# Products nobody reads, ahead of a kernel's prologue and behind each level's block in it

## What is computed

```python
# 1: 8 heads of 48 channels, a state of 48 x 48 per head
for t in range(S):
    cur = einsum('bhd,bhe->bhde', u * k_t, v_t)
    y[t] = einsum('bhd,bhde->bhe', r_t, state + cur)
    state = w_t[..., None] * state + einsum('bhd,bhe->bhde', k_t, v_t)
# 2: x is y as (4, 768, 384)
u  = x + (relu(x.T @ w_tok1) @ w_tok2).T          # mixing over tokens, 768 -> 256 -> 768
x2 = u + relu(u @ w_ch1) @ w_ch2                  # 384 -> 1536 -> 384
# 3
gate = sigmoid(causal 5-tap convolution of x2 along the tokens)
out  = (gate * (x2 @ w_val)) @ w_out              # 384 -> 384 -> 384
```

## Time and profile before

| | us |
|---|---|
| median of 3 runs | 733.45 |
| lowest and highest | 733.14, 733.71 |
| profiled execution | 737.69 |
| its span, first to last instruction | 736.0 |
| TensorE (PE) busy in the span | 680.0 |
| VectorE (DVE) busy | 407.7 |
| ScalarE (ACT), GpSimd (POOL) busy | 200.5, 102.4 |
| mean granted TensorE clock | 0.939 |

### The profile page before, as it was taken

How to read it: one execution, slowest core, us unless ns; L and a number is a source line. 1 busy time by engine, 2 the same in 40 slices (tenths; PEclk the granted TensorE clock), 3 DMA queues, 4 the chain that set the end, 5 groups by cost and what they waited for, 6 DMA issues and landing times.

```text
span 736.0 us, 26444 instructions
## 1 busy us (share of the span) xinstructions
PE 680.0 (92%) x12244; PEld 652.6 (89%) x12244; DVE 407.7 (55%) x624; ACT 200.5 (27%) x366; POOL 102.4 (14%) x139
## 2 busy tenths in 40 slices
PE   4558888999999999999999999999999999999995
PEld 3458878998989999989989999999989998999995
DVE  2749727639476548437485638429476534252524
ACT  2220340422423313311323313312323223131322
POOL 6121561130200200020210300030300100000000
PEclk9655578999999999998999999999999999999998
DMA  9594245250050320060050230040000000000000
GB/s 146 106 154 94 68 99 117 83 90 11 6 99 10 56 55 24 3 88 3 3 88 24 35 76 23 3 67 3 3 24 3 2 22 22 1 2 1 22 22 22
DMA packets 111357, 32.77 MB, mean 45 GB/s; under 512 B 104080, under 2 KB 110224, under 8 KB 111248
## 3 DMA queue, kind: packets, MB, share of 16 engines
q1 hardware_dynamic: 107792, 26.37, 21.0%
q10 hardware_dynamic: 3456, 4.72, 1.8%
HBM read 26.35 MB, written 4.72 MB: 42 GB/s over the span
## 4 chain that ended last, share of the span: by engine, by line
PE 69%; DVE 17%; SPq 4%; issue 4%; ACT 4%; DMA 1%; DVEq 0%; ACTq 0%
PE ps L733 66%; DVE gate L702 4%; DVE rk L572 4%; DVE at L625 3%; PE ps L755 3%; SPq L336 2%; SPq L323 2%; ACT x2s L454 1%; ACT gate L537 1%; DVE wp L572 1%; DMA nat<-in_k_dram 1%; DVE xf L679 1%; ACT hid L521 1%; DVE xf L683 1%; DVE us L664 1%
## 5 line engine op out<-in xcount | busy, mean ns | idle before, releaser
L733 PE MATMUL ps<-hid,ch 128*128 128x256 f32 x1296 | 172.1, 287 | 0.0
L733 PE MATMUL ps<-us,ch 128*128 128x256 f32 x1296 | 170.6, 286 | 1.5 <-DVE us L664 0.8
L733 PEld LDWEIGHTS ps<-us,ch 128*128 128x128 f32 x1296 | 160.0, 189 | 6.2 <-DVE us L664 2.0
L733 PEld LDWEIGHTS ps<-hid,ch 128*128 128x128 f32 x1296 | 160.9, 190 | 1.5
L651 DVE SCALAR_TENSOR_TENSOR hid<-ps,hid 128x512 fp32r<-128x512 f32 x72 | 50.0, 694 | 127.9 <-ACT hid L521 127.6
L572 DVE TENSOR_TENSOR rk<-rk,wp 112x1024 f32<-112x1024 f32 x72 | 89.6, 1244 | 45.3 <-PE ps L733 45.2
L733 PE MATMUL ps<-rk 48*64 48x32 f32 x4608 | 95.4, 237 | 19.1 <-DVE at L625 9.0
L733 PEld LDWEIGHTS ps<-rk 48*64 48x64 f32 x4608 | 88.3, 155 | 27.3 <-issue 13.4
L521 ACT ACTIVATE hid<-ps 128x512 fp32r<-128x512 f32 x72 | 42.8, 595 | 160.3 <-PE ps L733 160.3
L702 DVE SCALAR_TENSOR_TENSOR gate<-xf,cw,gate 128x256 f32<-128x256 f32 x144 | 74.7, 566 | 4.4 <-ACT gate L537 3.5
L625 DVE COPY_PREDICATED at<-mask,ps 128x512 f32<-128x512 uint8 x72 | 65.4, 908 | 0.0
(11 more groups left out here) (71 smaller groups left out, 619.1 us busy)
## 6 DMA issues: line engine op xcount, KB each, us to landing
nat<-in_r_dram SPq DMA_DIRECT2D x24, 192.0 KB, 4.0
nat<-in_k_dram SPq DMA_DIRECT2D x24, 192.0 KB, 5.0
nat<-in_w_dram SPq DMA_DIRECT2D x24, 192.0 KB, 5.1
vs<-in_v_dram SPq DMA_DIRECT2D x96, 48.0 KB, 2.5
out_dram<-gate ACTq DMA_DIRECT2D x24, 192.0 KB, 2.0
gate<-in_moe_w_ch_dram SPq DMA_DIRECT2D x6, 384.0 KB, 3.6
xf<-in_moe_w_ch_dram SPq DMA_DIRECT2D x6, 384.0 KB, 4.0
gate<-in_moe_w_tok_dram SPq DMA_DIRECT2D x2, 384.0 KB, 5.2
```

Of the source, the lines that this page charges most:

```text
L733: return nc.tensor.matmul(out, lhsT, rhs, start=start, stop=stop, skip_group_check=True, **kw)
```

## The change

A function `keep_clock` issues four products, one in each quarter of the array. Stationary is a 64x64 part of the identity matrix, moving are 128 of its columns, and the results go to columns 0 to 127 of banks 0 and 1, which hold nothing at that time: the first product of the dense stages writes there anew, after the last of them. It is called 16 times as soon as the identity matrix is there, ahead of the first transposes, and once behind every L block (six levels, not F) of super-units 0 to 2. These are 34 calls and 136 products. No wait and no increment is added or moved, and no other engine's work.

```diff
+IDLE_COLS, FIRST_IDLE = 128, 16
...
+            def keep_clock():
+
+                for two in range(2):
+                    for par in range(2):
+                        rows, turn = slice(par * CH, (par + 1) * CH), slot(par, 2 * two)
+                        mm(ps[turn * CH:(turn + 1) * CH, RING + par, 0:IDLE_COLS], ident[rows, 0:CH],
+                           ident[rows, 0:P].unsqueeze(1).to_broadcast([CH, IDLE_COLS // P, P]), True)
...
                     scores(s, bank, CH // 2, lambda rows, ph: r_sides[home(s)][rows, ph * CH:(ph + 1) * CH]
                            .rearrange("p (n two i) -> p n two i", two=2, i=m)[:, :, 1], lev_done[m])
+                    if s < SUPERS:
+                        keep_clock()
...
             pe.wait_ge(ident_done, 1)
+            for _ in range(FIRST_IDLE):
+                keep_clock()
```

## The result

| | before | change |
|---|---|---|
| median of 9 runs, us | 733.45 | 737.91 |
| lowest, highest | 732.93, 735.2 | 733.77, 740.58 |
| profiled execution, us | 737.69 | 738.54 |
| its span, us | 736.0 | 736.8 |

The ratio of the change to the kernel before is 1.0045, with a 95% interval from 1.0024 to 1.0065: slower, by 1.8 to 4.8 us. The medians stand 4.5 apart. The forecast was 3.9, at 737.3. Ratios leave out executions over 1.5% above the fastest of their kernel; of all kernels in this document only e3 had such executions, three of twelve.

A forecast was written before the change was run, and what follows sets the result against it. The prediction took the prologue as bound by SyncE's DMA issue, then mostly VectorE with TensorE even at half clock, then TensorE. Terms 1.0 + 2.4 + 0.5 gave 3.9 us slower, 737.3 us, range 730.0 to 740.5.

The forecast's parts named there:

- a delay at L16:2 arrives whole at the end: At VectorE's multiplication for L16:2, lag of 1.0 + 2.4 us arrives whole and is counted in full in the time.
- The signs named beforehand: Profile after: clock 0.50 from 52 to 97 us, saturated blocks 2.3 us apart, VectorE waiting from about 72, dense products about 4 later.
- The start costs nothing: 16 groups ahead of the first transposes, covered by SyncE's issue until 36.15 us and a load: nothing; 3 to 5 us uncovered.
- The two groups at 46 to 48: Two groups after the blocks at 46.3 to 48.3 us, where TensorE then has nothing until 52.2: no cost.
- Six groups, 1.0 us of lag: Between 52.2 and 67.3 us, 2.9 us of groups against 2.0 us of TensorE idle: 1.0 us lag, bounds 0 and 2.9.
- the gap would be swallowed by slower issue: A 0.82 us TensorE idle before 63.61 us, put down to issue, which slower issue may swallow.
- Five groups, 2.4 us: Behind the five saturated blocks, before T:0: 5 x 0.49 = 2.4 us; VectorE's lag soaks up the first three groups.
- The group behind L32:2, 0.5 us: The group after L32:2 stands in the stage where TensorE is the chain and costs 0.5 us.
- The cold case: The prologue's clock stays at half despite the groups: 3.9 us slower, 737.3 us, spread 735 to 740.5; chance 0.53.
- The reason I gave: Prologue clock: a group is only 0.49 of each 2.34 us, the rest being products of a kind that did not suffice.
- Rival 1: Groups lift the clock from some point after 52 us and hold it to 96: 3 us saved, 730.4 us; chance 0.25.
- Rival 3: A half-clock stretch in the dense part vanishes or appears, 3 to 5 us either way, on top of others; no separate chance.

The follow-up runs named there:

- e3: The change with groups of 512 columns in place of 128, 4 at the start and 18 behind blocks; ratio to the kernel before 1.0029.
- e5: Groups of 128 columns only behind the five blocks of the saturated stretch, none at the start; ratio to the kernel before 0.9979.
- e6: Groups of 128 columns only behind the six blocks ahead of the saturated stretch, none at the start; ratio to the kernel before 0.9960.
- e12: 24 groups at the start and none behind blocks; ratio to the kernel before 0.9994.
- e1: The change without the groups behind the blocks, only the 16 at the start; ratio to the kernel before 0.9997.
- e4: The change with groups of 32 columns in place of 128, 64 at the start and 18 behind blocks; ratio to the kernel before 1.0079.
- e2: The change without the groups at the start, only the 18 behind the blocks; ratio to the kernel before 1.0052.
- e10: The change with 22 groups at the start in place of 16, all 18 behind blocks kept; ratio to the kernel before 1.0043.
- e7: Groups of 512 columns only behind ten blocks from L2:2 to L32:2, none at the start; ratio to the kernel before 1.0101.

## Why the prediction was right, and where its sum was off

**Sign and size.** Slower by 3.9 us was forecast; 1.8 to 4.8 was measured. That the forecast lies so close is in part luck: of its terms one was too high, one cost was missing, and the step on which it rests, that a delay at L16:2 arrives whole at the end, failed in e5, e6 and e12. The runs show that the loss comes with the groups behind the blocks; by what path it reaches the end they do not show.

**The signs named beforehand.** The profiled execution was to come to 741.6 us and came to 738.54. The blocks stand 2.15 apart, not 2.3. VectorE was to be idle before its multiplications from about 72 us and waits from 79.64 on. The first dense product is 3.4 us late (116.59 against 113.18), where about 4 was said.

**The start costs nothing.** Right, by e1. The groups took 6.02 us rather than 7.8. With 64 groups (e4) the load came late, and the stage began 3.9 us later than before; whether through them is open.

**The two groups at 46 to 48.** Not run alone. In the change L4:1 follows an idle spell of 3.0 us (3.9 before), so they lie in idle time.

**Six groups, 1.0 us of lag.** In the profile of the change L4:2 starts 27.0 us behind the transposes, against 26.1 before (67.29 - 41.22): 1.0 us. In e2 it is 28.4, 2.3 more than before, beside issue gaps of 1.14 and 0.85 us inside L1:2 and L2:2 (the change has 0.58). In e6, which has these six alone, it is 26.7, 0.6 more, and VectorE's multiplication for L4:2 is not late at all. So the lag of TensorE was of the forecast's order. But VectorE's lateness at L4:2 (0.4 us in the change, 1.3 in e2, 2.2 in e10) goes with where the gaps of issue fall, and e12 has 1.9 without these groups. That the gap would be swallowed by slower issue held only in part.

**Five groups, 2.4 us.** Mis-sized. They cost 0.33 each, 1.6 in all. I scaled the length of the F block, 1.96 us from its first start to its last end, but what a block costs in a row of blocks is the distance to the next start. In the kernel before, the next block starts 1.74 us behind that F block (28.87):

```profile
30.61 1.88 PE L733 MATMUL ps<-rk 48*64 48x32 f32 x64
```

16/64 of 1.74 is 0.44, and 0.43 is what a group took alone. The further 0.1 is hidden behind a block: the weight loads of the next block start under the group's products (68.51, with the group at 68.26 to 69.03). The consequence stood in the change: VectorE's slack took up the first ones, and L16:2 came 2.4 us late in the change (3.4 forecast), 4.1 in e2 and 4.7 in e10.

**The group behind L32:2, 0.5 us.** VectorE's multiplication for L32:2 is 3.1 us late in the change (46.2 against 43.1 behind the transposes), so 0.6 was added already between L16:2 and L32:2, where I had nothing. It is made up of the multiplication for L16:2, 1.6 longer beside GpSimd's subtraction, and of L32:2's own products, ready 0.96 sooner with the short rise of the clock. In e2, without the rise, 1.1 was added there. What lies beyond L32:2 varies by more than this term from kernel to kernel, and it was not tested alone.

**The clock.** The cold case came: 0.50 from 52.2 to 76.5. After that it rose for 3.4 us, which shortened L32:2 by up to 0.96 and was then lost in the idle spell in T:1. The reason I gave, that the rest of the mix is of a kind that did not suffice, is weaker than it looked: that rise came with only small products and groups since 47 us, and in e3 the clock rose, in e7 it did not, with the same mix. Nor was it so that each rise before came with transposes or 128x384 products: the one at 336.0 us came with 128x256 products. The sentence of the Trainium skill ("TensorE: Matmul & The Clock Gate", "Why this matters for your kernels") that I set against the row fares as it did: TensorE busy 9.20 of 9.20 us at 0.50 again, and 9.00 of 9.00 in e7.

**Rival 1** was priced at 730.4 if the clock rose. e3 shows the full clock from 63 to 94 without that gain, though with wider groups; the time expected from the TensorE pieces of the chain went into gaps of issue. So the rival's price was too high where its condition was met. **Rival 3** is what separated the profiles: the half-clock stretch at 330 was there in one and not in the other.

**What was not foreseen:** that a few groups (e5, e6) leave the whole kernel no slower although they delay L16:2 by over 1 us. The chain from L16:2 to the dense work is looser than my sum had it, and a delay of 1 to 2 us there need not arrive. Whether it is the 2.4 to 4.7 us at L16:2 that arrive in the change, e2 and e10, or something else that the 18 groups bring, is open.

## What to carry to other kernels

Filler work for the clock is not free where an in-order engine has no room: find the stretch in which it runs back to back, and count what stands behind the filler, not the block ahead of it. Take its price from distances between starts, not from the length of a block. Ask also what the delayed engine will then run beside. Test that the clock does rise before counting on it, with several executions, since one mix rose in one kernel and not in another. And before two profiles are compared, compare a stretch that lies far behind the change; here 2.6 of 4 us hid in it.

## What the runs showed of the hardware

- At half clock a group of four products in the four quarters nets 0.17 us with 32 columns, 0.33 with 128, 1.59 with 512, behind a block of 64-column weights; alone, back to back, one of 128 columns takes 0.43, and 0.22 at full clock.
- The same multiplication of VectorE (112x1024, float32) beside the same subtraction of GpSimd (128x768) took 1.22 us and GpSimd 3.43 in the kernel before, 2.82 and 1.80 with the change.
- Full clock on small products can be worth little: e3 had it for 30.7 us, and TensorE stood for 5.9 us in gaps inside blocks between 77 and 96.
- Those gaps, where they occur, fall at fixed counts of TensorE's instructions, steps of 254, in all kernels, with about one transfer of 16384 bytes for each step; moving the work by 128 instructions gave no gain that could be repeated.
